# A chain of decayed attention, a top-2 mixture of experts and a gated layer: who gathers and combines the last stage's first block, and how its weights are loaded

## What is computed

```python
# attention with a decaying state, 4 x 8 heads, 768 steps, 48 wide
state = f[:, :, t, :, None] * state + np.einsum('bhd,bhe->bhde', k[:, :, t], v[:, :, t])
y[:, :, t] = np.einsum('bhd,bhde->bhe', q[:, :, t], state)
# mixture of experts over the 3072 rows of y (384 wide): 8 experts, two chosen a row
noisy_logits = x @ w_gate + np.log1p(np.exp(x @ w_noise)) * noise
for e in range(E):
    for k in range(2):
        mask = top2[:, k] == e
        h = np.maximum(x[mask] @ w1[e], 0.0)           # 384 -> 1024
        out[mask] += top2_w[mask, k, None] * (h @ w2[e])   # 1024 -> 384
# gated layer, 384 -> 1536 -> 384
xn = x / np.sqrt(np.mean(x * x, axis=-1, keepdims=True) + 1e-06) * rms_g
g = xn @ w_gate
out = g * (1.0 / (1.0 + np.exp(-g))) * (xn @ w_val) @ w_out
```

## Time and profile before

| | us |
|---|---|
| median of three runs | 1277.01 (1275.15 to 1278.94) |
| the profiled execution: time | 1272.26 |
| the profiled execution: span from first to last instruction | 1270.6 |
| TensorE busy (matmuls) | 1200.3, 94% |
| VectorE busy | 685.8, 54% |
| ScalarE busy | 491.0, 39% |
| GpSimd busy | 473.8, 37% |

### The profile page before, as it was taken

The page is one execution under the profiler, slowest core; times in us unless marked ns, Lnnn a source line. Parts: engine busy times, 40 slices in busy tenths (PEclk is TensorE's granted clock), DMA queues, the critical chain, the costliest instruction groups (busy, mean ns, idle before and its releaser), DMA issues.

```text
span 1270.6 us, 26415 instructions
## 1 busy us (share of the span) xinstructions
PE 1200.3 (94%) x8577; PEld 1109.0 (87%) x8578; DVE 685.8 (54%) x1274; ACT 491.0 (39%) x1033; POOL 473.8 (37%) x425
## 2 busy tenths in 40 slices
PE   4999999999999999999999992899999999999997
PEld 4777887878879999999999992899999999999997
DVE  7888898886334444444444440444454444444433
ACT  3656666655224333333333341333232323232321
POOL 8368787654625526254364256201010101010000
PEclk9999999999999999999999996899999999999999
DMA  6234433255377787878877862101010101010000
GB/s 221 84 93 130 135 115 115 85 184 212 84 235 212 236 227 233 249 214 242 240 223 233 241 200 76 51 25 56 1 57 19 38 19 38 19 37 19 0 20 19
DMA packets 96177, 156.89 MB, mean 123 GB/s; under 512 B 37728, under 2 KB 71776, under 8 KB 95584
## 3 DMA queue, kind: packets, MB, share of 16 engines
q1 hardware_dynamic: 84384, 107.81, 27.2%
q0 software_dynamic: 11712, 47.98, 12.8%
HBM read 103.52 MB, written 52.23 MB: 123 GB/s over the span
## 4 chain that ended last, share of the span: by engine, by line
PE 46%; POOL 20%; issue 14%; DMA 13%; DVE 4%; ACT 2%; POOLq 0%; DVEq 0%; SPq 0%; ACTq 0%
PE pD L1989 12%; PE pA L1989 12%; PE pA L2003 8%; DMA stage<-w 7%; POOL we L755 6%; PE pA L1694 5%; PE pS L2003 4%; POOL we L753 3%; DMA stage<-w_val 2%; DMA stage<-w_gate 2%; DMA stage<-w_out 2%; POOL stage L764 1%; POOL qk L650 1%; DVE W L1188 1%; POOL fT L631 1%
## 5 line engine op out<-in xcount | busy, mean ns | idle before, releaser
L1883 PE MATMUL pD<-we,xsH 128*128 x612 | 189.5, 391 | 0.0
L1630 DVE TENSOR_TENSOR gs<-pD,sig 128x384 f32<-128x384 f32 x96 | 53.5, 558 | 192.1 <-ACT sig L1121 192.1
L840 POOL DMA_INDIRECT pair<-y_sorted,y_row x48 | 46.1, 961 | 287.6 <-DVE z L1610 271.9
L1694 PE MATMUL pA<-W 64*128 64x128 f32 (+3 forms) x1920 | 137.7, 284 | 14.9 <-DVE W L1188 12.1
L1694 PEld LDWEIGHTS pA<-W 64*128 64x128 f32 (+3 forms) x1920 | 113.7, 172 | 33.9 <-DVE W L1188 17.2
L1883 PEld LDWEIGHTS pD<-we,xsH 128*128 128x128 f32 x612 | 114.1, 188 | 22.1 <-issue 0.2
L1121 ACT ACTIVATE sig<-pD 128x384 f32<-128x384 f32 x96 | 47.2, 491 | 204.1 <-PE pA L1989 204.0
L1912 PE MATMUL pA<-we,hidH 128*128 (+1 forms) x464 | 118.7, 336 | 1.8 <-issue 1.0
L1883 PE MATMUL pD<-we,xsL 128*128 x306 | 120.0, 392 | 0.0
L1188 DVE TENSOR_TENSOR W<-W,prods 128x512 f32<-128x512 f32 (+1 forms) x120 | 101.4, 851 | 23.8 <-PE pA L1694 21.9
L1368 DVE STREAM_TRANSPOSE pA<-hidP 128x512 f32<-128x512 f32 x98 | 64.6, 705 | 84.5 <-DMA hidP<-hid_rows 84.4
(11 more groups left out here) (262 smaller groups left out, 2731.4 us busy)
## 6 DMA issues: line engine op xcount, KB each, us to landing
hid_rows<-hid SPq DMA_DIRECT2D x49, 512.0 KB, 3.0
hidP<-hid_rows SPq DMA_DIRECT2D x196, 128.0 KB, 3.3
stage<-w POOLq DMA_DIRECT2D x48, 384.0 KB, 4.1
qk<-qk_t SPq DMA_DIRECT2D x24, 512.0 KB, 3.7
y_sorted<-yo SPq DMA_DIRECT2D x55, 192.0 KB, 3.5
xs<-x_sorted SPq DMA_DIRECT2D x200, 48.0 KB, 2.1
fT<-f_t SPq DMA_DIRECT2D x12, 512.0 KB, 4.1
vN<-v_n SPq DMA_DIRECT2D x24, 256.0 KB, 2.7
```

What stands on the lines that cost most here:

```text
L1630: dve.tensor_tensor(gs[:], pD[:, f % 2 * 512:f % 2 * 512 + TT], sig[f % 2][:], ALU.mult).then_inc(s_u, 1)
L1694: ins = pe.matmul(pA[par][keys, s, c * P:(c + 1) * P], both[r, 1, c, keys], both[r, 0, c], start=True, stop=True)
L1883: ins = pe.matmul(hidden_bank(t, h), (xsL if a else xsH)[t.par][:, k * P:(k + 1) * P], we[:, bass.ds(at + (b * WE + k * F + h * HF), HF)], ...
```

## The change

- GpSimd takes over the first block's gather and combine. It waits for the stores of the used slots alone (the count comes from `ends`, times 16, through a register), gathers into z_first and two other buffers, multiplies by the shares with tensor_scalar and adds with tensor_tensor. Five gathers are issued ahead of the first combine; the sixth follows it, since its buffer is that of the first.
- ScalarE's squares and roots of the first block wait for all three combines and write to buffers of their own (ms_first, rms_first); VectorE only divides. The root's table is loaded before the last slot's copy in place of after it.
- The later blocks' gathers start after all 55 stores and after the first block's transposes (`s_tz`).
- The last stage's weights are loaded with two pieces in flight (`in_turns`), on two semaphores in alternation.
- To make room, the slots have two x buffers in place of four and one yo in place of two; the loads and stores of SyncE wait and are ordered accordingly.

```diff
-        xs = [sb(f"xs{i}", [P, DM]) for i in range(4)]
+        xs = [sb(f"xs{i}", [P, DM]) for i in range(2)]
+        first_at = where[0]
+        xs += [sb(f"xs{i}", [P, DM]) for i in (2, 3)]
+        where[0] = first_at
+        z_first = sb("z_first", [P, TS, DM])
+        second = [sb("second0", [P, DM]), zero]
...
-        yo = [sb(f"yo{i}", [P, DM]) for i in range(2)]
+        yo = sb("yo", [P, DM])
...
+        def xs_of(t):
+            return xs[t.c] if early(t) else xs[t.par]
...
             def store_rows(t):
                 wait_alone(sp, s_yo, t.times(1, 1))
-                sp.dma_start(y_sorted[bass.ds(t.times(P), P), :], yo[t.par][:]).then_inc(s_ys[t.par], 16)
+                if t.c >= 1:
+                    wait_alone(sp, s_ys, t.times(16))
+                sp.dma_start(y_sorted[bass.ds(t.times(P), P), :], yo[:]).then_inc(s_ys, 16)
...
             wait_alone(sp, s_tx, 1)
             load_rows(Tile(4))
-            for n in (1, 2, 3):
-                wait_alone(sp, s_tx, n + 1)
-                load_rows(Tile(n + 4))
-                store_rows(Tile(n))
+            wait_alone(sp, s_tx, 2)
+            load_rows(Tile(5))
+            store_rows(Tile(1))
+            store_rows(Tile(2))
             wait_alone(sp, s_tx, 5)
+            load_rows(Tile(6))
+            store_rows(Tile(3))
+            wait_alone(sp, s_tx, 6)
+            load_rows(Tile(7))
+            store_hidden(Tile(5))
+            wait_alone(sp, s_tx, 7)
             load_rows(Tile(8))
-            store_hidden(Tile(5))
...
                     if (t + 4).before(SLOTS):
-                        wait_alone(sp, s_tx, t.times(1, 1))
+                        wait_alone(sp, s_tx, t.times(1, 3))
                         load_rows(t + 4)
...
+            def in_turns(to, fr, n):
+                for p in range(PIECES3):
+                    s = (s_stage1, s_stage2)[p % 2]
+                    if p >= 2:
+                        pool.wait_ge(s, landed3(n) + 16 * (p // 2))
+                    c = slice(p * PIECE, (p + 1) * PIECE)
+                    pool.dma_start(to[:, c], fr[:, c]).then_inc(s, 16)
+                pool.wait_ge(s_stage1, landed3(n + 1))
+                pool.wait_ge(s_stage2, landed3(n + 1))
...
-            in_pieces(stage3, w_gate2, s_stage1, landed3(0))
-            pool.wait_ge(s_stage1, landed3(1))
+            in_turns(stage3, w_gate2, 0)
...
+            def take_first(j, k, to):
+                pool.indirect_dma_start(
+                    out=to, out_offset=None, in_=y_sorted[:, :],
+                    in_offset=bass.IndirectOffsetOnAxis(ap=y_row[:, j, k:k + 1], axis=0)).then_inc(s_pair[j], 16)
+
+            def combine_first(j):
+                own, other = z_first[:, j], second[j % 2][:]
+                pool.wait_ge(s_pair[j], 32)
+                pool.tensor_scalar(own, own, share[:, j, 0:1], None, ALU.mult).then_inc(s_first, 1)
+                pool.tensor_scalar(other, other, share[:, j, 1:2], None, ALU.mult).then_inc(s_first, 1)
+                pool.wait_ge(s_first, FIRST * j + 2)
+                pool.tensor_tensor(own, own, other, ALU.add).then_inc(s_first, 1)
+
             pool.wait_ge(s_yrow, 10)
-            for t in range(NT2):
-                if t == 1:
-                    pool.wait_ge(s_first, FIRST_SUM[-1])
-                elif t:
+            stored = pool.value_load(rows_stored_i[0:1, 0:1], min_val=16, max_val=16 * SLOTS)
+            wait_alone(pool, s_ys, stored)
+            take_first(0, 0, z_first[:, 0])
+            take_first(0, 1, second[0][:])
+            take_first(1, 0, z_first[:, 1])
+            take_first(1, 1, second[1][:])
+            take_first(2, 0, z_first[:, 2])
+            combine_first(0)
+            pool.wait_ge(s_first, FIRST)
+            take_first(2, 1, second[0][:])
+            combine_first(1)
+            combine_first(2)
+
+            pool.wait_ge(s_ys, 16 * SLOTS)
+            pool.wait_ge(s_tz, KC)
+            for t in range(1, NT2):
+                if t > 1:
                     pool.wait_ge(s_z, (t - 2) * ZS + 2 * TS)
...
             def take_rows(t):
                 act.wait_ge(s_g2, t.times(1, 2))
-                if t.c >= 2:
-                    act.wait_ge(s_ys[t.par], t.over(2, 16))
-                act.copy(yo[t.par][:], y_bank(t)).then_inc(s_yo, 1)
+                if t.c >= 1:
+                    act.wait_ge(s_ys, t.times(16))
+                act.copy(yo[:], y_bank(t)).then_inc(s_yo, 1)
...
+                else:
+                    act.preload_act_table_set("sqrt_and_others")
                 take_rows(t)
...
-            act.wait_ge(s_g2, SLOTS + 1)
...
             for j in range(TS):
-                first_mean_square(j)
+                act.wait_ge(s_first, FIRST * TS)
+                if j >= 2:
+                    act.wait_ge(s_rms, 2 * j - 3)
+                act.activation(second[j % 2][:], z_first[:, j], ACT.Square,
+                               accum_out=ms_first[:, j:j + 1]).then_inc(s_rms, 1)
+                act.wait_ge(s_rms, 2 * j + 1)
+                act.activation(rms_first[:, j:j + 1], ms_first[:, j:j + 1], ACT.Sqrt, scale=1.0 / DM,
+                               bias=eps[:]).then_inc(s_rms, 1)
...
+            dve.tensor_scalar(rows_stored_i[:], ends[0:1, E - 1:E], 16.0, None, ALU.mult)
...
-            first_combine(0)
-            first_combine(1)
-            first_norm(0)
-            first_combine(2)
-            first_norm(1)
-            first_norm(2)
+            for j in range(TS):
+                dve.wait_ge(s_rms, 2 * j + 2)
+                dve.reciprocal(inv_first[:, j:j + 1], rms_first[:, j:j + 1]).then_inc(s_normed, 1)
+                dve.wait_ge(s_normed, 2 * j + 1)
+                dve.tensor_scalar(z_first[:, j], z_first[:, j], inv_first[:, j:j + 1], None,
+                                  ALU.mult).then_inc(s_normed, 1)
```

More of the change, by code:

```diff
@@ L186, in program @@
         eps = sb("eps", [P, 1])
+        ms_first = sb("ms_first", [P, TS])
+        rms_first = sb("rms_first", [P, TS])
+        inv_first = sb("inv_first", [P, TS])
         zero = sb("zero", [P, DM])
@@ L215, in program @@
         hidden_ends_i = sb("hidden_ends_i", [1, E], I32)
+        rows_stored_i = sb("rows_stored_i", [1, 1], I32)
         last = sb("last", [1, 1])
@@ L383, in program @@
         s_hp = sem("s_hp")
-        s_ys = [sem(f"s_ys{i}") for i in range(2)]
+        s_ys = sem("s_ys")
         s_tx = sem("s_tx")
@@ L397, in program @@
         s_first = sem("s_first")
+        s_normed = sem("s_normed")
         s_rms = sem("s_rms")
@@ L494, in program @@
         ZS, MS = 8, 4
-        FIRST_SUM, FIRST_NORM = (2, 4, 8), (6, 10, 12)
+        FIRST = 3
         RV, RQ, RA, PL = 7, 3, 4, 5
@@ L597, in _ @@
             store_hidden(Tile(6))
-            wait_alone(sp, s_tx, 6)
+            wait_alone(sp, s_tx, 8)
             load_rows(Tile(9))
@@ L770, in landed3 @@
             def landed3(n):
-                return landed1(E - 1) + 16 * PIECES3 * n
+                return landed1(E - 1) + 16 * PIECES3 // 2 * n
+            def in_turns(to, fr, n):
[7 more added lines that the diff above has]
+                pool.wait_ge(s_stage2, landed3(n + 1))
             def load_expert(e):
@@ L824, in _ @@
             pool.wait_ge(s_last, 2)
[L825 to L826 removed]
+            in_turns(stage3, w_out2, 2)
             for high, c in ((outHa, slice(0, OUT_A * DM)), (outHb, slice(OUT_A * DM, F2C * DM))):
                 split(high[:], outL[:, c], stage3[:, c], s_last)
[L830 to L836 removed]
+            def take_first(j, k, to):
[9 more added lines that the diff above has]
+                pool.tensor_tensor(own, own, other, ALU.add).then_inc(s_first, 1)
+            pool.wait_ge(s_yrow, 10)
+            stored = pool.value_load(rows_stored_i[0:1, 0:1], min_val=16, max_val=16 * SLOTS)
[14 more added lines that the diff above has]
+                if t > 1:
                     pool.wait_ge(s_z, (t - 2) * ZS + 2 * TS)
@@ L1584, in _ @@
             slots(dve, slot)
-            def first_combine(j):
-                dve.wait_ge(s_pair[j], 32)
-                dve.tensor_scalar(z[:, j], pair[:, j, 0], share[:, j, 0:1], None, ALU.mult).then_inc(s_first, 1)
-                dve.wait_ge(s_first, FIRST_SUM[j] - 1)
-                dve.scalar_tensor_tensor(out=z[:, j], in0=pair[:, j, 1], scalar=share[:, j, 1:2], in1=z[:, j],
-                                         op0=ALU.mult, op1=ALU.add).then_inc(s_first, 1)
-            def first_norm(j):
-                dve.wait_ge(s_rms, 2 * j + 2)
-                dve.reciprocal(inv[:, j:j + 1], rms[:, j:j + 1]).then_inc(s_first, 1)
-                dve.wait_ge(s_first, FIRST_NORM[j] - 1)
-                dve.tensor_scalar(z[:, j], z[:, j], inv[:, j:j + 1], None, ALU.mult).then_inc(s_first, 1)
             def combine(t, j):
@@ L1857, in turn_rows @@
                 for k in range(KC):
-                    ins = pe.transpose(pX[:, k * P:(k + 1) * P], chunk(xs[t.c % 4][:], k), ident[:])
```

(7 more changed lines are left out.)

20 lines of the change are left out of this document (5 added, 15 removed).

## The result

The change makes the kernel faster, by 1.3%, at the time predicted: a median of 1260.07 us over four runs (1257.75 to 1261.85) against 1276.09 us over four (1275.15 to 1278.94) for the kernel before on the same chip, ratio 0.987 [0.9844, 0.9896] (in brackets the 95% interval). The forecast was 1260.3.

What follows compares the result with a forecast made beforehand. GpSimd's chain of loads, splits and gather was taken to bound the first wide matmul. Loads save 26.0 us; after the gather, combines and squares it moves from 799.96 to 783.3: 1277.0 - 16.7 = 1260.3 us, range 1254 to 1267.

Steps and rivals of the forecast that it cites:

- The loads: Last stage's three weight loads on GpSimd's queue: two pieces in flight take 17.4 us each, 52.2 for 78.2, saving 26.0.
- check by capacity: Weight loads: with 0.46 of the DMA engines left to GpSimd's queue, a load would take 19.6 us; 17.4 was taken.
- the pieces share: Rival on the weight loads: the second piece only takes from the first, loads stay 78.2 us, kernel 1286.3; chance 0.07.
- The rule on two half transfers: Weight loads: a skill page says two half transfers serialize on the same 16 engines and are not worth splitting.
- The new wait costs nothing: First gather: the 52nd slot's store lands at 756.7, before GpSimd comes at 758.9, with 2.2 us to spare.
- the slots are slowed: Rival: some six slots take 1.5 us more each, gather at 762.1, first matmul 786.1, kernel 1263.1; chance 0.13.
- signs of being wrong: A piece with two in flight over 7 us, TensorE gaps between 663 and 745, or ScalarE store waits in the slots.
- GpSimd's combine: First block on GpSimd: 1.1 us per tensor_scalar, 0.9 per tensor_tensor, 3.3 per combine; the last ends at 776.8.
- GpSimd's one-input work is fast: Rival on the combine: six operations 0.65 us shorter each, first matmul 779.4, kernel 1256.4 or 1254.2; chance 0.22.
- the clamp's row: Basis for GpSimd's tensor_scalar: 1,024 elements at 2.8 us give 1.04 for 384; the cast's row would give 0.45.
- The rest: After the combines: 2.9 us of ScalarE squares and roots, 3.56 to the first wide matmul at 783.3; nothing later changes.
- early start: First gather waits only for the 52 used slots' stores of 55, and starts at 759.3 instead of 784.92.

Runs made afterwards that it cites:

- the second profile: The changed kernel run once more with no edit, for another profile of it; median 1260.13 us, 0.9859 of the kernel before.
- its second profile: The kernel before the change run once more with no edit, for another profile of it; median 1279.26 us, ratio 1.0005.

## Why the prediction was right, step by step

**The loads: right, a little undersized.** 52.2 us was forecast (three times 17.4); 55.9 and 53.6 were measured, and 52.9 to 57.2 in the nine profiles with two pieces in flight (mean 54.7). The reasoning (a further piece adds its service, not its latency) held beyond two: by it six in flight would take 4.3 + 5 x 1.5 = 11.8 us, and 11.5 to 13.0 were measured. The prediction's check by capacity left GpSimd 0.46 of the engines; its queue took 0.437 in the first load with two pieces, but 0.598 with six, where the slots' queue gave up the difference. The rival *the pieces share* fell. The rule on two half transfers that the prediction set beside it did not carry over to these pieces, which are columns of one matrix and had been loaded one after another: 55.9 us for 78.2. The rival's price was good all the same: loads of 80.7 us cost 8.0 us over the kernel before on that chip, forecast 9.3.

**The new wait costs nothing: half right.** The step had GpSimd at 758.9 and the 52nd store at 756.7. GpSimd was done at 760.75, but in the first profile the store was there only at about 765, for 4.44 us of wait; in the second there was no wait. In the second profile GpSimd itself came only at 765.7. So the gather stood at 765.19 and 765.89 for 759.3 forecast. The cause in the first profile is what the rival *the slots are slowed* named, and there it went further than the rival did (gather at 762.1, first wide matmul at 786.1). From the 45th slot's copy to the 52nd's it took 58.3, 59.6 and 58.7 us in the three profiles with one piece in flight (mean 58.8), and 58.4 to 65.7 us, mean 61.9, in the nine with two. The chain of waits of the change shows where that execution, the slowest of the nine here, lost part of it: an x load of 6.75 us, its transpose, and behind them the 2.85 us gap of TensorE shown above, a step for which the prediction had given the x loads no cost at all.

```profile
704.55 6.75 DMA xs<-x_sorted
...
711.33 0.71 DVE pX L1413
```

So two pieces in flight delay the slots by 3 us on average and by 0 to 7 in one execution. The prediction kept this as a rival at 0.13; it is a spread rather than a case. The two kernels with six pieces had 59.4 and 60.0 in this stretch, but their first load lies wholly ahead of it. With that load taken in, from the 40th slot's copy to the 52nd's, it is 99.8 to 101.8 us in the three profiles with one piece in flight, 100.3 to 106.6 in the nine with two (mean 103.7), and 106.0 and 107.4 with six. ScalarE's timeline of the change with six pieces has the 40th, the 44th and the 45th copy:

```profile
654.22 0.47 ACT L1076 COPY yo<-pA 128x384 f32<-128x384 f32 x1
...
689.55 0.47 ACT L1076 COPY yo<-pA 128x384 f32<-128x384 f32 x1
700.84 0.48 ACT L1076 COPY yo<-pS 128x384 f32<-128x384 f32 x1 [0.45 <-DMA y_sorted<-yo]
```

These two lose 5 to 6 us against one piece, more than the mean with two. GpSimd was waiting for the 52nd slot's store there, so what the slots lose comes straight off the gather's start, and six pieces gain nothing, with either engine combining.

Of the prediction's signs of being wrong, the gaps of TensorE between 663 and 745 us came about (2.85 and 1.59 us), and the last piece of w_val took some 8 us (issued at 703.50, the cast behind it starts at 711.65) while its load as a whole took 18.4. ScalarE's waits for stores came to 0.7 us in all. In its text on this rival, 756.7 with six slots at 1.5 us less 4.4 of slack gives 761.3 for the store and not 761.7, which moves nothing.

**GpSimd's combine: near, a little undersized.** Forecast 1.1 for a tensor_scalar and 0.9 for a tensor_tensor; by shape they measured:

```profile
L869 POOL TENSOR_SCALAR z_first<-z_first,share 128x384 f32<-128x384 f32 x3 | 3.8, 1257 | 0.1
...
L872 POOL TENSOR_TENSOR z_first<-z_first,second 128x384 f32<-128x384 f32 x2 | 2.0, 1002 | 0.2
```

From the first gather to the last combine's end 18.1 us, forecast 17.5. The rival *GpSimd's one-input work is fast* fell: the operation with one tensor input was the slower of the two, 3.3 ns an element against 2.6. The choice of the clamp's row over the cast's was right. The rule of the Trainium skill's GPSIMD Engine Reference (4.1, Engine selection) on one-input work does not hold for this tensor_scalar; its advice to give elementwise work to VectorE does, where a tile of that size took 0.42 + 0.62 = 1.04 us in place of 3.6.

**The rest: right.** From the last combine to the first wide matmul 6.2 us, forecast 6.5; after it nothing changed. Half clock on return was met: 0.50 from 781 us on, and both kernels' first wide matmul takes 0.69 us.

**What the sum did not say.** 16.7 us was forecast and 16.0 measured, but the two parts are not what they seem. By the prediction's own figures, the loads alone bring GpSimd to 758.9, where it would wait for all 55 stores. The last copy ends at 769.57; with a store's landing behind it and 15.0 us from there, the first matmul falls near 788, so 12 of the 16.7 were the loads' own by this estimate, and the rest of the bundle was to bring 4.8 us more: some 13.8 for the early start (769.57 + 3.5 - 759.3), less 9.0 for GpSimd's combine (24.0 for 15.0). The experiments are clearer still: 0.9861 and 0.9875 for the loads alone, 0.987 and 0.9859 for the whole. The 9.0 was right (9.3 measured). The early start was sized too large, since the gather came at 765.19 and not at 759.3: its 11 us and GpSimd's 9 nearly cancel, and what is left is within the noise. The prediction compared the bundle with the kernel before and never each part with the bundle less that part; the total came out right, and the better version, with the combine left on VectorE, went unnamed.

The small errors fell on one side within the change (the first gather at 765.19 for 759.3, 4.44 of the 5.9 us being the wait; 0.6 on the combine; the first wide matmul at 789.50 for 783.3) and were balanced by the profile of before, which was a quick execution: its second profile has 805.59 for 799.96. The forecast set the gain against the median, not against that execution, and a gain of 15.4 to 16.0 is close to 16.7. That the median came within 0.3 us of the forecast is therefore luck in part. The saving on the loads, the main term, was shown; the 6 us by which the changed kernel's first wide matmul was missed are hidden by a median of before that lies above its first profile.

## What to carry to other kernels

Price each part of a bundle against the bundle without it: here the loads gave all that the whole gave, and moving the combine to GpSimd, with the squares behind all three tiles, cost 9 of the 11 us that the earlier start brought. An early start pays by the engine that does the work, so keep the gather on the queue that is free and the arithmetic on the fast engine, tile by tile. Where one piece after another is loaded beside traffic that uses half of the DMA engines, a second piece in flight takes a third off the load; going on to six shortened the loads by another third here and gained nothing, since GpSimd then waited for the slots, which had become slower. Take several profiles of each kernel where their steps vary by more than the effect: one pair showed 10.5 us here for a gain of 16.

## What the runs showed of the hardware

A 384 KB piece on GpSimd's queue cost 4.3 to 4.5 us with one in flight, 3.1 with two (18.6 us a load) and 2.0 with six (12.3 us a load), next to the slots' traffic. The DMA engines' busy share tells little of how much more goes through. In the first load it was 0.87 at 255 GB/s with one piece in flight, 0.98 at 301 in the change's first profile with two, and 0.94 at 310 with six.

TensorE's clock outlasted a short pause. In the kernel with VectorE's combine the granted clock was still 1.00 when the first transposes came after 3.14 us of idle time, and the first of them took 0.30 us, for 0.45 in the change after 8.33 us, where the clock had fallen to 0.50 during the pause. It fell in the next pause, of 2.16 us, and the first wide matmuls ran at half clock as in all the others.

```profile
778.00:779.60 1.60, 1.46 (x9) 0.93 (x9) 1.00 (x4) 0.49 (x3) 0.00 (x0) 1.00 0.00 0
779.60:782.00 2.40, 0.24 (x2) 0.17 (x2) 1.67 (x3) 2.38 (x4) 1.24 (x2) 0.51 0.00 0
782.00:785.00 3.00, 3.00 (x10) 3.00 (x11) 0.00 (x0) 0.32 (x1) 2.39 (x3) 0.50 0.61 154
```
